# TensorE's transposes of h placed ahead of the w_out products in the last five slots of a pipelined attention and feed-forward kernel

## The reference

```python
# q, k, v: (2, 8, 576, 64)
scores = scale * np.matmul(q, k.transpose(0, 1, 3, 2))
kth = np.partition(scores, -32, axis=-1)[..., -32:-31]
scores = np.where(scores >= kth, scores, -1e9)
attn = softmax(scores)                      # with + 1e-9 in the denominator
x = (attn @ v)  ->  (1152, 512)
x = ((x @ w_a) * (x @ w_b)) @ w_out         # d_ff = 1536
for e in range(4):                          # w1: (4, 512, 1024), w2: (4, 1024, 512)
    out += p[:, e:e+1] * (np.maximum(x @ w1[e], 0.0) @ w2[e])
```

## Time and profile before

| | us |
|---|---|
| median of 3 executions | 841.15 |
| the three executions | 841.04, 841.15, 841.94 |
| time of the profiled execution | 841.94 |
| its span in the trace | 840.1 |
| PE busy in the span | 800.0 (95%) |
| DVE busy | 459.9 (55%) |
| ACT busy | 387.7 (46%) |
| POOL busy | 298.6 (36%) |

### The profile page before, as it was taken

How to read it: one execution, slowest core, us unless ns; L and a number is a source line. 1 busy time by engine, 2 the same in 40 slices (tenths; PEclk the granted TensorE clock), 3 DMA queues, 4 the chain that set the end, 5 groups by cost and what they waited for, 6 DMA issues and landing times.

```text
span 840.1 us, 13049 instructions
## 1 busy us (share of the span) xinstructions
PE 800.0 (95%) x4949; PEld 707.0 (84%) x4949; DVE 459.9 (55%) x904; ACT 387.7 (46%) x721; POOL 298.6 (36%) x270
## 2 busy tenths in 40 slices
PE   5469899999999999999999999999999999999998
PEld 3247778888888888888989989899899899898996
DVE  6999998989999999996124212112122122121121
ACT  6677778787777777776534002311032010230110
POOL 2868775555545454545330000620026000440000
PEclk9978999999999999999999999999999999999999
DMA  9450684475545754545779400230004100000001
GB/s 239 124 151 5 235 270 163 151 223 173 190 151 188 252 189 151 176 152 176 254 274 321 153 1 0 101 101 1 1 1 150 51 1 1 1 1 38 13 26 38
DMA packets 71663, 102.59 MB, mean 122 GB/s; under 512 B 32560, under 2 KB 48944, under 8 KB 71600
## 3 DMA queue, kind: packets, MB, share of 16 engines
q1 hardware_dynamic: 70544, 101.48, 37.3%
q10 hardware_dynamic: 1056, 0.26, 0.2%
HBM read 88.36 MB, written 13.37 MB: 121 GB/s over the span
## 4 chain that ended last, share of the span: by engine, by line
PE 84%; DVE 6%; ACT 3%; POOL 2%; issue 2%; DMA 2%; SPq 0%; ACTq 0%; POOLq 0%; DVEq 0%
PE ps L638 24%; PE ps L658 23%; PE ps L537 14%; PE ps L522 8%; PE ps L450 4%; PE ps L486 4%; PE ps L463 3%; DVE m L912 2%; DVE work L918 2%; PE ps L495 2%; DMA wo<-wo_d 2%; DVE work L906 1%; POOL p_sb L1049 1%; DVE m L902 1%; ACT s_sb L721 1%
## 5 line engine op out<-in xcount | busy, mean ns | idle before, releaser
L805 ACT ACTIVATE h_hi<-ps 128x384 fp32r<-128x384 f32 x96 | 47.1, 491 | 269.7 <-PE ps L638 269.5
L912 DVE MAX8 m<-work 128x8 f32<-128x576 f32 x216 | 152.2, 746 | 0.0
L1105 POOL TENSOR_TENSOR w_lo<-w_raw,w_hi 128x2048 fp32r<-128x2048 f32 x12 | 55.1, 4617 | 244.4 <-ACT w_hi L801 244.4
L976 DVE SCALAR_TENSOR_TENSOR h_lo<-ps,h_hi 128x384 fp32r<-128x384 f32 x96 | 53.4, 558 | 156.6 <-ACT h_hi L805 156.5
L638 PE MATMUL ps<-x_hi,w_hi 128*128 128x384 f32 x384 | 129.0, 336 | 0.0
L638 PE MATMUL ps<-x_hi,w_lo 128*128 128x384 f32 x384 | 128.8, 336 | 0.0
L638 PE MATMUL ps<-x_lo,w_hi 128*128 128x384 f32 x384 | 128.8, 335 | 0.0
L658 PE MATMUL ps<-w_hi,h_hi 128*128 128x512 f32 x288 | 112.2, 390 | 0.0
L658 PE MATMUL ps<-w_hi,h_lo 128*128 128x512 f32 x288 | 112.2, 390 | 0.0
L658 PE MATMUL ps<-w_lo,h_hi 128*128 128x512 f32 x288 | 112.1, 389 | 0.0
L1049 POOL TENSOR_TENSOR p_sb<-s_sb,p_sb 128x576 f32<-128x576 f32 x72 | 102.0, 1434 | 18.9 <-ACT p_sb L727 18.9
(11 more groups left out here) (95 smaller groups left out, 1496.2 us busy)
## 6 DMA issues: line engine op xcount, KB each, us to landing
wo<-wo_d SPq DMA_DIRECT2D x96, 512.0 KB, 5.0
w_raw<-moe_w_in SPq DMA_DIRECT2D x16, 1024.0 KB, 7.1
wo_d<-wo SPq DMA_DIRECT2D x12, 512.0 KB, 3.9
w_raw<-moe_w_a_in SPq DMA_DIRECT2D x4, 768.0 KB, 4.9
w_raw<-moe_w_b_in SPq DMA_DIRECT2D x4, 768.0 KB, 4.9
wo_raw<-moe_w_out_in SPq DMA_DIRECT2D x12, 256.0 KB, 3.9
x_d<-x_hi_out SPq DMA_DIRECT2D x9, 256.0 KB, 2.9
x_d<-x_lo_out SPq DMA_DIRECT2D x9, 256.0 KB, 3.1
```

The source lines that it names most:

```text
L805: copy(h_hi[:, m, :], ps[:, UP + m % FREE_UP, 0:GN], ACT.Relu).then_inc(ac_r, 1)
L912: nc.vector.max(m8[:, par, i, 8 * r:8 * r + 8], work[:, i, :]).then_inc(ve_top, 1)
L976: nc.vector.scalar_tensor_tensor(h_lo[:, m, :], ps[:, UP + m % FREE_UP, 0:GN], 0.0, h_hi[:, m, :].bitcast(F32), ALU.max, ALU.subtract).the ...
L1105: nc.gpsimd.tensor_tensor(lo[:, s, :], raw[s][:], hi[:, s, :].bitcast(F32), ALU.subtract).then_inc(done, 1)
```

## The change

In slots 36 to 40 `h_transpose(u)` moves from behind `send(u - 1)` to ahead of it, so that all slots from 5 on have the same order. `u` is never None there, so the calls are the same in number. No other engine's program changes, and no wait is added or taken away; the transposes' waits (`po_h`, `ac_b`) now stand ahead of the nine matmuls of `send`.

```diff
@@ -579,12 +579,10 @@
                     pe.wait_ge(ac_k, KEYS1_BY[n])
                 if n + 1 < NP:
                     scores(n + 1)
-                if u is not None and n < NP:
+                if u is not None:
                     h_transpose(u)
                 if sent_of(n) is not None:
                     send(sent_of(n))
-                if n >= NP:
-                    h_transpose(u)
                 if m < PR:
                     pe.wait_ge(po_w, SLICES.index((0, m)) + 1)
                 if m % PR == 0:
```

## The result

| | before | changed |
|---|---|---|
| median, first comparison | 841.55 us | 850.6 us |
| single executions | 841.04 to 842.5 | 849.91 to 851.26 |
| ratio, with its 95% interval | | 1.0106 (1.0089 to 1.0124) |
| profiled execution: time, span | 841.94, 840.1 | 850.07, 848.3 |

The change costs 9.05 us on the medians. The forecast was 6.85 us and 848.0, with a range that ended at 850.3. The changed kernel's lines behind 587 have numbers that are lower by two: L636 is the experts' product that was L638, L1061 POOL's product that was L1063.

What follows compares the result with a forecast made beforehand. The prediction took TensorE's own work to bound the kernel; the slots' added shifts, 0.60 + 0.16 + 2.05 + 2.30 + 1.74 = 6.85 us, on the median 841.15 made 848.0 us, range 846.4 to 850.3.

Steps and rivals of the forecast that it cites:

- What bounds the kernel: Whole kernel: TensorE's own work bounds it, so time PE loses before 440 us is not made up later.
- Terms of the sum: Slots 36 to 40: transposes wait for POOL's product, adding 0.60, 0.16, 2.05, 2.30 and 1.74 us; chance 0.55.
- the late chunks of slots 39 and 40: Send's losses there on late chunks, about 1.0 and 0.36 us, would be covered by the new waits.
- the place of x2_low: POOL, slot 39: x2_low of tile 7, 2.03 us, runs ahead of the product; PE idles 3.14 us.
- a free POOL: Slot 39: with POOL free altogether, idle falls by 1.24 us, giving 846.8; shorter-detour rival, chance 0.11.
- SP and the early transposes at nothing: Slots 36 to 40: SP's chunk loads shift with send, and earlier transposes help nobody; both counted as 0 us.
- The clock: Rival, slots 38 to 40: TensorE's clock falls in the gaps, 1.7 us per fall; chance 0.25.
- 849.7: Forecast time in us with one clock fall behind the gap of slot 39, 848.0 plus 1.7.
- Faster: Rival, slots 36 to 40: h ready when the w_b product ends, so idle and chunk losses vanish: 839.8; chance 0.02.
- nothing: Rival, slots 36 to 40: send's matmuls go ahead of the waiting transposes, 841.15; no effect or within 0.2%, chance 0.03.
- late chunks: Rival, send(34) behind slot 40: chunks come up to 1.9 us late, 849.9 at most; chance 0.04.

Runs made afterwards that it cites:

- the trace without a fall: The changed kernel measured a second time, nothing altered, against the kernel before: 849.01 us, ratio 1.009; its stage from slot 35 to the experts took 55.67 us.
- slot 39's gap alone: The kernel before with the transposes ahead of send in slot 39 only: 844.68 us, ratio 1.0039 to the kernel before.
- the first trace: Profiled execution of the changed kernel in its first measurement against the kernel before: 850.07 us; stage from slot 35 to the experts 58.36 us.
- third trace: Trace of the changed kernel measured a third time, nothing altered, against the kernel before: median 849.04 us, ratio 1.0095; stage 58.75 us.
- the longer gap: The changed kernel with POOL's product of unit 33 computed twice: 850.99 us, ratio 1.0115 to the kernel before; with useless matmuls filling the gaps 849.35 us, ratio 1.0086.

## Why the prediction was right or wrong

**What bounds the kernel.** Right. The stretch behind the slots took 402.17 and 402.20 us; what the slots lost was lost for good.

**Terms of the sum.** Right in mechanism and nearly in size. Start of w_a against the kernel before, from the transposes of slot 35 on: slot 36 0.59 (forecast 0.60), slot 37 0.72 (0.76), slot 38 2.68 (2.81). For slots 39 and 40 the trace without a fall must be taken; it gives 4.93 (5.11) and 6.63 (6.85), and 6.55 to the experts. The idle times read 1.71 and 2.99 where I wrote 1.90 and 3.14, because the profile counts idle time from the modelled end of a matmul and I counted from the next possible start, 0.17 us ahead of it. That the late chunks of slots 39 and 40 would be covered was right, and so was the place of x2_low; moving it gave 1.2 us, the bound of 1.24 that the prediction had for a free POOL.

**SP and the early transposes at nothing.** Right: in all three traces of the changed kernel PE's only waits from 384 to 455 us are those for POOL's product, none for a chunk and none for h_out.

**The clock.** Here the prediction failed: it put the fall of the clock at nothing in the sum, and gave it too small a chance and too small a price. I gave the fall 0.25, on the ground that PE is full around the new gaps while it was not near 43 us. That ground does not hold: with slot 39's gap alone, 2.68 us between full stretches, the clock fell. The granted clock of 1.00 from 397 to 446 us that the prediction named is there in one of three traces of the changed kernel, the two others show falls, and eight of its 14 executions lie in the upper heap.

The price was taken from one fall, 3.4 us at the low level and 1.7 us lost. Behind slot 39 the first trace shows 6.9 us at the low level, which cost 9.24 - 6.55 = 2.69; half of the 6.9 would be 3.4, but for 0.8 us of them PE stood anyway. The third trace shows two falls of 3.4 us, which cost 3.08 together. On the base of the first comparison, and with the fall of its trace, the account nearly closes: 841.55 + 6.55 + 2.69 = 850.8, where 850.6 was measured. One row was too little for a price. Near 43 us, where all kernels run the same program, the clock was low for 3.4 us in the trace before, but for 6.8 in the second and in the third trace of the changed kernel (a mean of 0.66 over the 10 us from 39 to 49).

The first comparison had all its executions in the upper heap (849.91 to 851.26), above 849.7 and mostly above the 850.3 at which the range ended; the two others had medians of 849.0, inside it. That all five of the first were in the upper heap was in part luck, unless chips differ. The range had to hold 6.85 + 3.1, about 851; over the 14 executions the two cases came about equally often, if the heaps are taken for them.

The Trainium skill's rule that an idle TensorE falls back to the low clock (TensorE: Matmul & The Clock Gate, Part 1), which I put at 0.25, agrees with the falls in so far as each followed a wait of PE; but in one trace the same gaps did not bring one, and in some the clock went down only when PE was working again.

**Faster, nothing, late chunks.** None came about. That there was something to gain from the late chunks was right, but by moving the transfers, not the transposes: the kernel that does so, and has send first in slot 35 too, is faster by 1.45 us on the medians; in the traces it gains 1.4 us, with POOL's order 1.9.

## What to carry to other kernels

Look at what stands between an engine's output and its own use of it by way of other engines, and count it off against the work placed between. Here the way over ACT and POOL is 1.7 us past the point where PE goes on, and send, 2.1 us that need none of it, covers it; an order that costs little where a weighted_sum ends the slot before (0.5 us in slots 36 and 37) costs the full way where none does. When a change opens gaps like these in a stretch that TensorE bounds, put the fall of its clock in as a case of its own, price it from more than one trace, and let the range hold two. Matmuls of no use, sized to end before the awaited signal, kept the clock up here. And before crediting a removed wait, ask who was late behind it: in slot 39 it was POOL.

## What of the hardware was not expected

In slots 35 to 40 the clock fell behind gaps of 1.83, 2.68, 2.99, 3.00 and 4.06 us, and not behind others of 2.99 (in another execution of the same kernel), 1.70 to 1.80 and 1.09. The 1.83 is a case apart, since its gap began less than 5 us after the end of another fall. The fall need not begin in the gap: in the traces with the 2.99 and the 4.06 it did, while behind the 1.83, 2.68 and 3.00 it came 0.3 to 1.3 us after PE had started again. All low stretches there lasted 3.4 or 6.8 to 6.9 us. Single times of the changed kernel on one chip spread by 3.5 us, while those of the kernel before spread by 1.6 us in the same comparison. And 34 matmuls of no use in the gaps cost 0.1 us; with these, or 40 behind the longer gap, the clock is at 1.00 in all three traces.

The record of the clock can miss a low stretch. At 29.6 us of the trace before it says 1.00, but four transposes take 1.12 us there, against 0.66 at 38.1 us; in the second trace of the changed kernel they take 1.12 too, and the record says 0.50. So it is safer to check a clock of 1.00 by the duration of a known piece, as above by the 0.55 of the transposes and the 2.48 to the w_a product.

What stays open: whether a gap brings a fall in a given execution could not be told from its length alone, why one fall lasted 6.9 us and others 3.4, and whether chips differ in how often it comes.
